# A second half-batch of banded attention moved to TensorE blocks, and the low parts of the first weights moved off TensorE

## The chip, the cores and the metric

The kernel runs on one core of a Trainium2 chip. Its time is the time that the device takes for one execution, in microseconds (us). The engines are named as the profile names them: PE is TensorE (PEld its weight loads), DVE is VectorE, ACT is ScalarE, POOL is GpSimd, SP is SyncE, which here issues most transfers (DMA).

## What is computed

An attention layer (4 batches, 8 heads, 576 tokens, head size 64) is followed by two feed-forward layers on its 2304 x 512 output, all in float32:

```python
q_d = q.reshape(B, H, Sd, factor, D).mean(axis=3)      # factor 4: also k_d, v_d
out_d = sm_attn(q_d, k_d, v_d)                          # full softmax attention on 144 groups
out_up = np.repeat(out_d, factor, axis=2)
mask = np.abs(pos[:, None] - pos[None, :]) < factor     # a band of 7 keys for each query
scores = np.where(mask, scale * np.matmul(q, k.transpose(0, 1, 3, 2)), -1000000000.0)
out_local = np.matmul(softmax(scores), v)               # softmax with 1e-9 in the divisor
x = (out_up + out_local).transpose(0, 2, 1, 3).reshape(B * S, H * D)
h = x @ w_in;  g = s * np.maximum(h, 0.0) ** 2 + b;  x = g @ w_out
h = x @ w_in2; g = h - np.tanh(h);                   out = g @ w_out2
```

## The kernel before

**Tiles and subs.** The first feed-forward layer works on 8 tiles of 288 tokens; tile j is the output of half a batch, which the code calls sub j (batch j // 2, half j % 2). For each tile and each of 16 slices f of the hidden layer PE has a group `hidden1(j, f)` of 12 matmuls into a bank of `hid`, and three slices later a group `output1(j, f)` of 12 matmuls into `acc`. Twelve, because every float32 operand is split in a high part (a rounded copy, made by ACT) and a low part (what the copy left out, made by subtraction), and high x high, low x high and high x low are summed over 4 blocks. The second layer has 6 tiles of 384 tokens and follows when the first is done.

**Weights.** w_in and w_out come in four 1 MB loads each (`load_w1a`, `load_w1b`). ACT makes the high parts (L1207). The low parts of the 32 pieces are made by POOL (L873), and for every fourth piece by PE: two matmuls, the raw piece by the identity and the high part by minus the identity, into a bank of `pa` (L1416, L1417), from which ACT copies the result (L1214).

**The band.** Sub 0 is computed in blocks by PE before the first tile ("dense": transposes L1429 and L1434, scores L1447, probabilities turned L1458, values L1475, with the masks and the softmax on DVE and ACT); it uses `hid` and `acc` while these are still free. Subs 1 to 7 are computed by DVE: products of queries and shifted keys (L988), their sums (L997), the softmax (L1029 to L1045), products with the values (L1058), a tree of sums (L1066 to L1076) into `oloc`. PE transposes `oloc` (L1529) into `pa`, and DVE adds the coarse attention `up` and writes `xraw` (L1107 for sub 1, L1118 for later ones). ACT copies the high part `xh` (L1320), POOL subtracts for the low part `xl` (L878). Two tiles of x are held, so that sub j is written when tile j - 2 has been read.

**The coarse attention** of each batch (group sums by POOL and DVE, transposes L1408, scores L1488, turned probabilities L1499, `weigh` L1516) runs beside the tiles, on PE between the large groups.

**What sets the order.** A planner in the kernel (`Plan`) lists all steps with costs, ranks and dependences, plays them once, and so fixes one order for each engine; the engines then run their lists and wait for each other by semaphores. All side work of PE during the tiles goes through the two banks of `pa` in turn ("fills"): a fill waits until the bank's last content has been taken out (`s_free0`, `s_free1`), and the large groups that stand behind it in PE's list wait too.

Of the kernel before, what the change touches and what calls it, by code (L numbers as in the profile page):

```python
# [13 lines left out]
P = 128  # L14
# [50 lines left out]
assert BSTEP1 * (BLOCKS - 1) + BQ == NS and DKEY % 3 == 0  # L65
# [7 lines left out]
def low_maker(f, half):  # L73

    return ("POOL", "POOL", "POOL", "PE")[(f + half) % 4]
# [106 lines left out]
def plan():  # L182
# [14 lines left out]
    for f in range(FT):  # L197
        for half in range(2):
            after = [(("load_w1a", "load_w1b")[half], f // WGROUP)]
            if half and f >= WGROUP:  # L200
                after.append(("dense_values", NPAIR - 1))
            o.add("ACT", act(512), (2, f + 3 * half) if f + 3 * half > 3 else (1, 0, 5), ("w1_high", f, half), after)
            maker = low_maker(f, half)
            if maker == "PE":
                o.add("PE", 1.1, (0, 9, f), ("w1_rest", f, half), [("w1_high", f, half)], 0.5, fills=True)
                o.add("ACT", act(512), (0, 9, f), ("w1_low", f, half), [("w1_rest", f, half)],
                      empties=("w1_rest", f, half))
            elif maker == "DVE":
                o.add("DVE", add(512), (0, 0, 9), ("w1_low", f, half), [("w1_high", f, half)])
            else:  # L210
                o.add("POOL", pool(512), (1, 0, NLOAD + f + 3 * half), ("w1_low", f, half), [("w1_high", f, half)])


    o.add("SP", 2.4, (0, 0, 0, 0), ("load_dense_keys",), kbytes=700)
    o.add("SP", 1.8, (0, 0, 0, 1), ("load_dense_queries",), kbytes=600)
    o.add("SP", 3.0, (1, 0, 0), ("load_dense_values",), kbytes=700)
    o.add("POOL", 3.0, (0, 1), ("dense_mask",))
    for a in range(NPAIR):
        o.add("PE", 1.0, (0, 0, 30 + 0), ("dense_turn", a), [("load_dense_keys",), ("load_dense_queries",), ("identity",)]
# [3 lines left out]
        o.add("ACT", 0.8, (1, 0, 30 + 0), ("dense_queries", a), [("dense_turn", a)] + ring)  # L223
        o.add("PE", 1.5, (0, 0, 30 + 1), ("dense_scores", a), [("dense_keys", a), ("dense_queries", a)]
# [8 lines left out]
        o.add("PE", 2.4, (0, 0, 30 + 3), ("dense_values", a), [("dense_place", a), ("load_dense_values",)]  # L233
              + {1: [("dense_keys", 3)], 2: [("dense_queries", 3)], 3: [("dense_add", 0)]}.get(a, []))
        o.add("DVE", 0.55, (0, 0, 0), ("dense_add", a), [("dense_values", a), ("place_up", 0, a)])

# [4 lines left out]
    for b in range(BATCH):  # L241
        for n in range(NLOAD):
# [5 lines left out]
                  kbytes=384 if n < 6 else 160)  # L248
# [10 lines left out]
        for n in range(6):  # L259
# [4 lines left out]
            o.add("ACT", 0.75, (1, b, n), ("place_columns", b, n), [("transposes", b, n)],  # L264
                  empties=("transposes", b, n))
        for i in range(2 * NPAIR):
# [3 lines left out]
            if b == 0 and qh:  # L270
                after.append(("dense_add", NPAIR - 1))
            o.add("PE", 0.3, (0, b, 6 + 2 * i), ("scores", b, i), after, lead(b), fills=True)
# [4 lines left out]
            o.add("ACT", 1.0, (1, b, 6 + 2 * i), ("score_exp", b, i), after, empties=("scores", b, i))  # L277
            o.add("DVE", 0.2, (0, b, i), ("score_inverse", b, i), [("score_exp", b, i)], .8 if b else 0.6)
            o.add("ACT", 0.64, (1, b, 7 + 2 * i), ("score_scale", b, i), [("score_inverse", b, i)])
# [5 lines left out]
            o.add("PE", 0.3, (0, b, 7 + 2 * i), ("turn_probs", b, i), after, lead(b), fills=True)  # L285
            o.add("ACT", 0.34, (1, b, 8 + 2 * i), ("place_probs", b, i), [("turn_probs", b, i)],
                  empties=("turn_probs", b, i))
            if b == 0 or qh:
                w = i if b == 0 else hp
                after = [("place_probs", b, i), ("group_sums", b, 7 + 2 * hp)]  # L290
                if b:
                    after.append(("add_up", b * NSUB - 1, NPART - 1))
                o.add("PE", 0.4, (0, b, 8 + 2 * i), ("weigh", b, w), after, lead(b), fills=True)
                o.add("ACT", 0.22, (1, b, 9 + 2 * i), ("place_up", b, w), [("weigh", b, w)], empties=("weigh", b, w))


    for s in range(1, SUBS):
        b = s // NSUB
        for i, (kind, loads, kbytes) in enumerate((("load_queries", 4, 600), ("load_keys", 4, 1000),
                                                   ("load_values", 4, 1000))):  # L300
            user = "value_products" if kind == "load_values" else "key_products"
            rank = (0, b, 2 * (s % NSUB) + (i == 2), i) if s > 1 else (2, (1, 1, 4)[i], i)
            o.add("SP", 0.6 * loads, rank, (kind, s), [(user, s - 1, len(UNITS) - 1)] if s > 1 else [], kbytes=kbytes)
        for a, (h2, t0, nt) in enumerate(UNITS):
            o.add("DVE", add(nt * BAND * HD), (1, s, a), ("key_products", s, a),
                  [("load_queries", s), ("load_keys", s)] + ([("score_inverse", 0, NPAIR - 1)] if s == 1 else []),
                  takes="prod")
            o.add("DVE", dve(nt * BAND * HD), (1, s, a), ("key_sums", s, a),
                  [("key_products", s, a)] + ([("band_exp", s - 1)] if s > 1 and a == 0 else []), gives="prod")
        o.add("DVE", 0.95, (1, s, 4), ("band_max", s), [("key_sums", s, len(UNITS) - 1)] + (  # L310
            [] if s > 1 else [("masks",)]))
        o.add("ACT", 0.32, (0, b, s), ("band_exp", s),
              [("band_max", s)] + ([("value_products", s - 1, len(UNITS) - 1)] if s > 1 else []))
        o.add("DVE", 1.0, (0, s, 5), ("band_norm", s), [("band_exp", s)], .6)
        for a, (h2, t0, nt) in enumerate(UNITS):
            after = [("band_norm", s), ("load_values", s)]
            if s > 1 and a == 0:
# [1323 lines left out]
```

## Time and profile before

| what | value |
|---|---|
| median of 3 runs | 942.22 us (941.83 to 943.9) |
| the profiled execution, its own time | 940.56 us |
| its span in the trace | 938.5 us |
| mean granted TensorE clock | 0.987 of full speed |
| busy: PE, DVE, ACT, POOL | 96%, 56%, 46%, 34% |
| first matmul of tile 0, of tile 1, of tile 2 | 50.70, 125.59, 187.75 us |
| first matmul of the second layer | 534.44 us |
| read from memory, written | 55.40 MB, 9.44 MB |

Times in the trace count from the start of the span. The chain of waits follows the work that ended last back from the end, at each step to what released it. A row of a timeline has the start, the length, the engine, the line, the operation, the output and inputs by the program's names, the shape, and in brackets the idle time just before and what ended it.

### The profile page before, as it was taken

How to read it: one execution, taken by the hardware profiler on the slowest of the kernel's cores; microseconds unless marked ns; L12 is line 12 of the kernel's file. 1: busy time of each engine (PE TensorE's matmuls, PEld its weight loads, DVE VectorE, ACT ScalarE, POOL GpSimd, SP SyncE). 2: the span in 40 equal slices, each digit the busy share in tenths (PEclk: the TensorE clock that was granted, in tenths of full speed). 3: DMA queues.
4: the chain of work that ended last, by engine and by line, in shares of the span. 5: the costliest groups of instructions: out<-in, count | busy, mean ns of one | idle time of the engine just before them, and what ended most of it. 6: DMA issues, size and time to landing. Idle time of an engine off the chain costs nothing.

```text
span 938.5 us, 15072 instructions
## 1 busy us (share of the span) xinstructions
PE 897.9 (96%) x5763; PEld 836.5 (89%) x5763; DVE 522.8 (56%) x641; ACT 432.0 (46%) x1096; POOL 319.3 (34%) x298
## 2 busy tenths in 40 slices
PE   5798999998999899999999999999999999999997
PEld 4576899998999899999999999999999999999996
DVE  4779979999898999982002452332322323322321
ACT  3777485555655575536546642322322323222221
POOL 6678867997369942533222100000000000000000
PEclk9798999999999999999999999999999999999999
DMA  8992242443334331002113600100200200100101
GB/s 227 264 285 78 75 110 68 111 106 96 68 102 114 105 69 43 27 1 94 34 38 132 227 14 1 56 13 1 68 1 1 68 1 0 35 1 1 34 1 34
DMA packets 41785, 65.81 MB, mean 70 GB/s; under 512 B 10932, under 2 KB 22770, under 8 KB 41714
## 3 DMA queue, kind: packets, MB, share of 16 engines
q1 hardware_dynamic: 40466, 63.28, 24.5%
q10 hardware_dynamic: 1248, 1.57, 0.6%
q8 instruction: 46, 0.75, 0.3%
q14 instruction: 25, 0.20, 0.1%
HBM read 55.40 MB, written 9.44 MB: 69 GB/s over the span
## 4 chain that ended last, share of the span: by engine, by line
PE 76%; DVE 12%; issue 3%; ACT 3%; DMA 3%; SPq 2%; DVEq 0%; ACTq 0%
PE acc L1606 21%; PE hid L1588 21%; PE hid L1549 16%; PE acc L1569 15%; DVE prod L1058 3%; DMA wb_raw<-in_moe_w_out_dram 3%; DVE prod L1066 2%; DVE prod L1071 2%; DVE oloc L1076 1%; PE pa L1488 1%; DVE sc L997 1%; ACT pc L1250 1%; PE pa L1516 1%; SPq L748 1%; DVE own L1008 1%
## 5 line engine op out<-in xcount | busy, mean ns | idle before, releaser
L887 POOL TENSOR_TENSOR gl<-relu,gh 128x288 fp32r<-128x288 f32 x128 | 133.0, 1041 | 179.1 <-PE acc L1569 141.4
L1569 PE MATMUL acc<-gh,wbh 128*128 128x288 f32 (+1 forms) x512 | 155.9, 305 | 0.2 <-ACT ystage L1347 0.2
L1549 PE MATMUL hid<-xh,wah 128*128 128x288 f32 x512 | 154.7, 304 | 1.1 <-POOL wal L873 1.1
L1143 DVE TENSOR_TENSOR gdif<-hid,tanh 128x384 f32<-128x384 f32 x96 | 53.5, 557 | 182.8 <-ACT tanh L1370 182.8
L1569 PE MATMUL acc<-gl,wbh 128*128 128x288 f32 (+1 forms) x512 | 152.0, 297 | 0.0
L1569 PE MATMUL acc<-gh,wbl 128*128 128x288 f32 (+1 forms) x512 | 151.8, 296 | 0.0
L1549 PE MATMUL hid<-xh,wal 128*128 128x288 f32 x512 | 150.4, 295 | 0.0
L1549 PE MATMUL hid<-xl,wah 128*128 128x288 f32 x512 | 146.8, 294 | 0.0
L1370 ACT ACTIVATE tanh<-hid 128x384 f32<-128x384 f32 x96 | 47.2, 491 | 186.9 <-PE hid L1588 186.9
L1588 PE MATMUL hid<-x2h,wah 128*128 128x384 f32 x384 | 129.0, 336 | 0.8 <-DVE gdif L1143 0.8
L1588 PE MATMUL hid<-x2h,wal 128*128 128x384 f32 x384 | 129.0, 336 | 0.0
L1588 PE MATMUL hid<-x2l,wah 128*128 128x384 f32 x384 | 128.9, 336 | 0.0
L1329 ACT ACTIVATE relu<-hid 128x288 f32<-128x288 f32 x128 | 52.3, 408 | 144.7 <-PE hid L1549 129.5
L1606 PE MATMUL acc<-wbl,g2h 128*128 128x512 f32 x288 | 112.6, 391 | 0.0
L1606 PE MATMUL acc<-wbh,g2l 128*128 128x512 f32 x288 | 112.4, 390 | 0.0
L1606 PE MATMUL acc<-wbh,g2h 128*128 128x512 f32 x288 | 112.2, 390 | 0.0
L1549 PEld LDWEIGHTS hid<-xh,wah 128*128 128x128 f32 x512 | 96.4, 188 | 4.4 <-issue 1.4
L1569 PEld LDWEIGHTS acc<-gh,wbh 128*128 128x128 f32 x512 | 97.1, 190 | 2.7 <-issue 1.1
L1569 PEld LDWEIGHTS acc<-gh,wbl 128*128 128x128 f32 x512 | 97.0, 190 | 0.7
L1569 PEld LDWEIGHTS acc<-gl,wbh 128*128 128x128 f32 x512 | 97.0, 189 | 0.0
L1549 PEld LDWEIGHTS hid<-xh,wal 128*128 128x128 f32 x512 | 96.2, 188 | 0.7
L1549 PEld LDWEIGHTS hid<-xl,wah 128*128 128x128 f32 x512 | 94.9, 188 | 0.0
(133 smaller groups left out, 1591.5 us busy)
## 6 DMA issues: line engine op xcount, KB each, us to landing
wa_raw<-in_moe_w_in_dram SPq DMA_DIRECT2D x8, 1024.0 KB, 8.6
wb_raw<-in_moe_w_out_dram SPq DMA_DIRECT2D x8, 1024.0 KB, 11.4
kl<-in_k_dram SPq DMA_DIRECT2D x27, 240.0 KB
vl<-in_v_dram SPq DMA_DIRECT2D x27, 240.0 KB
x2T<-ystage SPq DMA_DIRECT2D x8, 576.0 KB, 3.1
x2raw<-x2T SPq DMA_DIRECT2D x6, 768.0 KB, 4.5
own<-in_q_dram SPq DMA_DIRECT2D x11, 384.0 KB
ql<-in_q_dram SPq DMA_DIRECT2D x28, 144.0 KB, 3.7
```

Source lines behind the costliest of these rows:

```text
L748: sp.dma_start(dval[0:BK, i, :, :], dram(v, BKEY0[i] * HD, [[HD, BK], [HSTEP, HEADS], [1, HD]])).then_inc(s_dval, 16)
L887: g.tensor_tensor(out=gl[:, turn % LRING1, 0:NS], in0=relu[:, f % 2, :], in1=gh[:, turn % GRING1, 0:NS].bitcast(F32), op=ALU.subtract).the ...
L1058: ve.tensor_tensor(prod[:, 0:nt, :, :], vv, pv, ALU.mult).then_inc(s_mul, 1)
L1066: ve.tensor_tensor(prod[:, 0:nt, 0:3, :], prod[:, 0:nt, 0:3, :], prod[:, 0:nt, 3:6, :], ALU.add).then_inc(s_tree, 1)
L1071: ve.tensor_tensor(pairs, pairs, others, ALU.add).then_inc(s_tree, 1)
L1143: ve.tensor_tensor(gdif[:, f % 2, :], hid[:, f % 2, 0:N2], tanh[:, f % 2, :], ALU.subtract).then_inc(s_dif, 1)
L1329: sc.activation(r, hid[:, f % 2, 0:n], ACT.Relu).then_inc(s_relu, 1)
L1370: sc.activation(tanh[:, f % 2, :], hid[:, f % 2, 0:N2], ACT.Tanh).then_inc(s_tanh, 1)
L1549: one = pe.matmul(dst, w[:, d, cols], x[:, j % XRING, d, :], start=i == 0, stop=i == len(products) - 1)
L1569: one = pe.matmul(acc[:, d, n], w[:, f, cols], g[:, turn % ring, n], start=(f == 0 and p == 0), stop=(f == FT - 1 and p == 2))
L1588: one = pe.matmul(hid[:, f % 2, 0:N2], w[:, d, f * P:(f + 1) * P], x[:, j % 2, d, :], start=(d == 0 and p == 0), stop=(d == KT - 1 and p = ...
L1606: one = pe.matmul(acc[:, i, :], g[:, f % GRING2, i * P:(i + 1) * P], w[:, f, :], start=(f == 0 and p == 0), stop=(f == FT - 1 and p == 2))
```

## The change

Sub 1 is now computed in blocks by PE as well ("late"), for four pairs of heads. Its loads take the place of sub 1's loads of queries, keys and values in SP's list: rows of 64 numbers (256 bytes), as for sub 0, where the loads before had runs of 576 and 960 numbers. For each pair PE has six fills: keys turned, queries turned, scores, probabilities turned in two parts, values. All go through the two banks of `pa`, and DVE and ACT take each out. Two of the 24 fills stand before tile 0, the others between the groups of tile 0. The late buffers lie where the band's buffers lie, so DVE's first band product (now of sub 2) and its loads wait for the last late steps. x of tile 1 is split pair by pair as it is finished.

PE makes no low parts of weights any more: of the pieces from the fourth turn on, DVE makes every other one and POOL the rest (`turn_of` is f + 3 x half, half 1 being w_out, and is also the order in which ACT makes the high parts). Several costs, ranks and leads of the planner are changed, and the mask of the blocks has a third part.

```diff
+LKEY0 = [BSTEP1 * i for i in range(BLOCKS - 1)] + [DKEY - BK]
+LPARTS = [(0, 3), (3, 2)]
+SB = NSUB
 def low_maker(f, half):
-    return ("POOL", "POOL", "POOL", "PE")[(f + half) % 4]
+    return ("POOL", "DVE")[(f + half) % 2] if turn_of(f, half) >= 3 else "POOL"
+def turn_of(f, half):
+    return f + LAG1 * half
...
-    lead = lambda b: 3 if b else 0.0
+    lead = lambda b, late=False: 3 if b > 1 else 1.5 if b else 1.0 if late else 0.0
...
-            o.add("SP", 0.6, (2, 2 * g + 3 * i), (kind, g), after, kbytes=680)
+            o.add("SP", 0.6, (2, 2 * g + 3 * i), (kind, g), after, kbytes=620)
...
+            o.add("DVE", add(512), (0, 0, 24), ("w1_low", f, half), [("w1_high", f, half), ("dense_add", NPAIR - 1)])
...
+    for i, (kind, kbytes) in enumerate((("load_late_keys", 600), ("load_late_queries", 590), ("load_late_values", 870))):
+        o.add("SP", (2.4, 1.8, 3.0)[i], (2, (1, 1, 4)[i], i), (kind,), kbytes=kbytes)
+    for a in range(NPAIR):
+        o.add("PE", 0.35, (0, 0, 20), ("late_turn", 1, a), [("load_late_keys",)] + first, late, fills=True)
+        o.add("DVE", 0.45, (0, 0, 20), ("late_keys", a), [("late_turn", 1, a)] + ring, 0.3, empties=("late_turn", 1, a))
+        o.add("PE", 0.35, (0, 0, 20), ("late_turn", 0, a), [("load_late_queries",)] + first, late, fills=True)
+        o.add("ACT", 0.85, (-1, 0, 20), ("late_queries", a), [("late_turn", 0, a)] + ring, empties=("late_turn", 0, a))
+        o.add("PE", 1.0, (0, 0, 21), ("late_scores", a), [("late_keys", a), ("late_queries", a)] ..., late, fills=True)
+        o.add("DVE", 1.6, (0, 0, 21), ("late_max", a), [("late_scores", a)] ..., 0.3, empties=("late_scores", a))
+        o.add("ACT", 0.5, (-1, 0, 21), ("late_exp", a), [("late_max", a)])
+        o.add("DVE", 1.2, (0, 0, 22), ("late_norm", a), [("late_exp", a)], 0.3)
+        for part, (i0, n) in enumerate(LPARTS):
+            o.add("PE", 0.11 * n, (0, 0, 22), ("late_probs", a, part), [("late_norm", a)] ..., late, fills=True)
+            o.add("ACT", 0.1 + 0.13 * n, (-1, 0, 22), ("late_place", a, part), [("late_probs", a, part)] ...)
+        o.add("PE", 0.9, (0, 0, 23), ("late_values", a), [("late_place", a, 1), ("load_late_values",), ...], late, fills=True)
+        o.add("DVE", 0.45, (0, 0, 19), ("late_add", a), [("late_values", a)], 0.3, empties=("late_values", a))
...
-    for s in range(1, SUBS):
+    for s in range(SB, SUBS):
...
+                after = [("late_values", NPAIR - 1) if kind == "load_values" else ("late_turn", 0, NPAIR - 1)]
...
+                if s == SB and a == 0:
+                    r, m = bank("late_values", NPAIR - 1)
+                    ve.wait_ge(s_full[r], m)
```

**ACT, just before the first tile.** `wah` and `wbh` are the high parts of w_in and w_out, `s_wa1`, `s_wb0` and so on the loads that they wait for (the number is that of the load of four slices), `xh` the high part of x, `s_dadd` sub 0's last additions, `dpT` sub 0's turned probabilities. Before:

```order
L1207 ACTIVATE wah<-wa_raw 128x4x128 [waits s_wa0]
L1207 ACTIVATE wbh<-wb_raw 128x512 [waits s_wb0]
L1207 ACTIVATE wah<-wa_raw 128x4x128 [waits s_wa1]
L1320 ACTIVATE xh<-xraw 128x288 [waits s_dadd]
L1214 ACTIVATE wbl<-pa 128x512 [waits s_full0]
L1214 ACTIVATE wal<-pa 128x4x128 [waits s_full1]
L1329 ACTIVATE relu<-hid 128x288 [waits s_h]
```

and after:

```order
L1353 ACTIVATE wah<-wa_raw 128x4x128 [waits s_wa1]
L1472 ACTIVATE xh<-xraw 128x288 [waits s_dadd]
L1343 ACTIVATE dpT<-acc 66x512 [waits s_dprob,s_dout]
L1345 ACTIVATE dpT<-acc 66x128
L1353 ACTIVATE wbh<-wb_raw 128x512 [waits s_wb1,s_dout]
L1472 ACTIVATE xh<-xraw 128x288 [waits s_dadd]
L1353 ACTIVATE wah<-wa_raw 128x4x128 [waits s_wa1]
L1353 ACTIVATE wbh<-wb_raw 128x512 [waits s_wb1]
L1353 ACTIVATE wah<-wa_raw 128x4x128 [waits s_wa2]
L1311 ACTIVATE lqT<-pa 64x5x60 [waits s_full1,s_lzero]
```

A high part from the second load of w_out (`s_wb1`) now stands ahead of the last `xh` of tile 0; the copies of PE's low parts are gone.

**PE, after the second `output1` group of tile 0.** `pc` and `pT` belong to the coarse attention, `lkT`, `lqT` and `lkey` to the late blocks. Before:

```order
L1516 MATMUL pa<-pT,vd 64x72 [waits s_free0,s_sums]
L1516 MATMUL pa<-pT,vd 64x72 x3
L1516 MATMUL pa<-pT,vd 64x72 [waits s_free1,s_sums]
L1516 MATMUL pa<-pT,vd 64x72 x3
L1416 MATMUL pa<-wb_raw,ident 128x512 [waits s_w1high,s_minus,s_free0]
L1417 MATMUL pa<-wbh,minus 128x512
L1416 MATMUL pa<-wa_raw,ident 128x512 [waits s_w1high,s_minus,s_free1]
L1417 MATMUL pa<-wah,minus 128x512
```

and after:

```order
L1698 MATMUL pa<-ident,pc 72x72 [waits s_pc,s_free0]
L1698 MATMUL pa<-ident,pc 72x72 x3
L1608 MATMUL pa<-lkT,lqT 128x66 [waits s_free1,s_free0]
L1608 MATMUL pa<-lkT,lqT 128x66 x4
L1597 MATMUL pa<-ident,lkey 128x97 [waits s_free0]
L1597 MATMUL pa<-ident,lkey 128x97 x2
L1748 MATMUL hid<-xh,wah 128x288 [waits s_relu,s_w1vlow]
```

The first pair's scores and the second pair's keys stand where the low parts stood, and a large group follows at once.

**DVE, where sub 2's band begins.** The first product of sub 2 is the row with `ql,kl`. Before:

```order
L1071 TENSOR_TENSOR prod<-prod 128x4x2x64 [waits s_tree]
L1076 TENSOR_TENSOR oloc<-prod 128x4x64 [waits s_tree]
L988 TENSOR_TENSOR prod<-ql,kl 128x2240 [waits s_red,s_kl,s_ql]
L997 TENSOR_REDUCE sc_72<-prod 128x35 [waits s_mul,s_bexp]
L1107 TENSOR_TENSOR xraw<-pa,up 128x4x16 [waits s_full1]
```

and after:

```order
L1065 TENSOR_TENSOR xraw<-pa,up 128x288 [waits s_full0,s_free1]
L1138 TENSOR_TENSOR own<-own 128x6x64 [waits s_stage1]
L1141 TENSOR_TENSOR ks<-own 128x192 [waits s_vpairs]
L1065 TENSOR_TENSOR xraw<-pa,up 128x288 [waits s_full0,s_free0]
L1118 TENSOR_TENSOR prod<-ql,kl 128x2240 [waits s_kl,s_ql,s_full0]
L1065 TENSOR_TENSOR xraw<-pa,up 128x288 [waits s_full0,s_free1]
```

It followed the last sums of sub 1, and now follows the third of the four late additions and waits (`s_full0`) for the values of the fourth pair on PE.

## Rows read from the trace of the kernel before

**Rows 1.** The page: PE's busy time, share and instructions, with the other engines'.

```profile
PE 897.9 (96%) x5763; PEld 836.5 (89%) x5763; DVE 522.8 (56%) x641; ACT 432.0 (46%) x1096; POOL 319.3 (34%) x298
```

**Rows 2.** The page: shares of the chain that ended last, by engine.

```profile
PE 76%; DVE 12%; issue 3%; ACT 3%; DMA 3%; SPq 2%; DVEq 0%; ACTq 0%
```

**Rows 3.** Windows: length; busy PE, PEld, DVE, ACT, POOL; clock, DMA share, GB/s.

```profile
50.70:125.59 74.89, 66.57 (x459) 59.57 (x457) 69.18 (x73) 51.79 (x144) 61.80 (x44) 0.95 0.46 128
125.59:187.75 62.16, 61.25 (x476) 58.25 (x475) 54.51 (x51) 39.67 (x121) 46.38 (x41) 1.00 0.42 109
...
427.37:478.64 51.27, 51.27 (x389) 51.27 (x387) 5.24 (x10) 27.75 (x64) 15.97 (x20) 1.00 0.18 59
```

**Rows 4.** Waits of PE from 50.7 to 125.6: in total, times, longest.

```profile
PE pa L1529 <- DVE oloc L1076: 4.7, 2, 3.7
PE pa L1488 <- DVE xraw L1107: 1.2, 1, 1.2
```

**Rows 5.** Windows of 10 us, columns as in rows 3.

```profile
0.00:10.00 10.00, 0.00 (x0) 0.00 (x0) 2.94 (x6) 1.59 (x2) 6.71 (x20) 1.00 0.79 180
...
80.00:90.00 10.00, 6.30 (x36) 5.04 (x35) 9.90 (x6) 7.85 (x17) 10.00 (x6) 0.90 0.20 68
90.00:100.00 10.00, 10.00 (x56) 8.85 (x55) 9.76 (x17) 3.06 (x8) 4.42 (x5) 0.76 0.26 86
```

**Rows 6.** Timeline of PE in tile 0: two low parts, and six transposes of sub 1.

```profile
80.05 1.02 PE L1416 MATMUL pa<-wb_raw,ident 128*128 128x512 f32 x2
...
81.15 1.02 PE L1416 MATMUL pa<-wa_raw,ident 128*128 128x512 f32 x2
...
108.74 0.85 PE L1529 MATMUL pa<-ident,oloc 128*128 128x128 f32 x6 [0.97 <-DVE oloc L1076]
```

**Rows 7.** Timeline of PE before tile 0: one pair of sub 0's blocks, step by step.

```profile
18.18 0.69 PE L1429 MATMUL hid<-ident,dkey 97*128 97x97 f32 x3
18.67 0.68 PE L1434 MATMUL hid<-ident,dqry 96*128 96x96 f32 x3
...
26.95 1.23 PE L1447 MATMUL acc<-dkT,dqT 128*128 128x66 f32 x10
28.01 0.71 PE L1458 MATMUL acc<-ident,dprob 128*66 128x128 f32 x5
...
29.14 0.80 PE L1475 MATMUL acc<-dpT,dval 66*64 66x57 f32 x20
```

**Rows 8.** Weights: the chain's first load, two issues, and their times to landing.

```profile
25.76 17.72 DMA wb_raw<-in_moe_w_out_dram
25.29 0.43 SPq L776 DMA_DIRECT2D wa_raw<-in_moe_w_in_dram  x1
37.80 0.54 SPq L788 DMA_DIRECT2D wb_raw<-in_moe_w_out_dram  x1
wa_raw<-in_moe_w_in_dram SPq DMA_DIRECT2D x1, 1024.0 KB, 14.8
wb_raw<-in_moe_w_out_dram SPq DMA_DIRECT2D x1, 1024.0 KB, 19.1
```

**Rows 9.** Timelines of ACT and POOL around the first matmul of tile 0.

```profile
43.51 0.63 ACT L1207 ACTIVATE wbh<-wb_raw 128x512 fp32r<-128x512 f32 x1 [1.16 <-DMA wb_raw<-in_moe_w_out_dram]
48.23 0.44 ACT L1320 ACTIVATE xh<-xraw 128x288 fp32r<-128x288 f32 x1 [0.35 <-DVE xraw L948]
50.16 0.80 POOL L878 TENSOR_TENSOR xl<-xraw,xh 128x288 fp32r<-128x288 f32 x1
```

**Rows 10.** Timelines of DVE and POOL: sub 2 from its first product to its x.

```profile
108.73 2.87 DVE L988 TENSOR_TENSOR prod<-ql,kl 128x2240 f32<-128x2240 f32 x1
114.10 1.87 DVE L1107 TENSOR_TENSOR xraw<-pa,up 128x64 f32<-128x64 f32 x10
177.00 0.40 DVE L1118 TENSOR_TENSOR xraw<-pa,up 128x128 f32<-128x128 f32 x1
179.96 4.91 POOL L878 TENSOR_TENSOR xl<-xraw,xh 128x288 fp32r<-128x288 f32 x4
```

More of the change, by code:

```diff
@@ L195, in plan @@
             after = [("dense_values", NPAIR - 1)] if i and 2 * g >= FT // WGROUP else []
-            o.add("SP", 0.6, (2, 2 * g + 3 * i), (kind, g), after, kbytes=680)
[L197 to L211, printed above, removed]
@@ L214, in plan @@
-    o.add("SP", 2.4, (0, 0, 0, 0), ("load_dense_keys",), kbytes=700)
-    o.add("SP", 1.8, (0, 0, 0, 1), ("load_dense_queries",), kbytes=600)
-    o.add("SP", 3.0, (1, 0, 0), ("load_dense_values",), kbytes=700)
+            o.add("SP", 0.6, (2, 2 * g + 3 * i), (kind, g), after, kbytes=620)
+    for f, half in sorted(itertools.product(range(FT), range(2)), key=lambda one: turn_of(*one)):
+        turn = turn_of(f, half)
+        after = [(("load_w1a", "load_w1b")[half], f // WGROUP)]
+        if half and f >= WGROUP:
+            after.append(("dense_values", NPAIR - 1))
+        if turn > 1:
+            after.append(("place_up", 0, NPAIR - 1))
+        o.add("ACT", act(512), (2, turn) if turn > 2 else (1, 0, 5), ("w1_high", f, half), after)
+        maker = low_maker(f, half)
+        if maker == "PE":
+            o.add("PE", 1.1, (0, 9, f), ("w1_rest", f, half), [("w1_high", f, half), ("hidden1", 0, 1)], 0.5, fills=True)
+            o.add("ACT", act(512), (0, 9, f), ("w1_low", f, half), [("w1_rest", f, half)],
+                  empties=("w1_rest", f, half))
+        elif maker == "DVE":
+            o.add("DVE", add(512), (0, 0, 24), ("w1_low", f, half), [("w1_high", f, half), ("dense_add", NPAIR - 1)])
+        else:
+            o.add("POOL", pool(512), (1, 0, NLOAD + turn), ("w1_low", f, half), [("w1_high", f, half)])
@@ L263, in plan @@
             o.add("PE", 0.35, (0, b, n), ("transposes", b, n), after, lead(b), fills=True)
-            o.add("ACT", 0.75, (1, b, n), ("place_columns", b, n), [("transposes", b, n)],
+            o.add("ACT", 0.75, (0 if b else -1, b, n), ("place_columns", b, n), [("transposes", b, n)],
                   empties=("transposes", b, n))
@@ L270, in plan @@
             if b == 0 and qh:
-                after.append(("dense_add", NPAIR - 1))
-            o.add("PE", 0.3, (0, b, 6 + 2 * i), ("scores", b, i), after, lead(b), fills=True)
+                after.append(("hidden1", 0, 0))
+            o.add("PE", 0.3, (0, b, 6 + 2 * i), ("scores", b, i), after, lead(b, qh), fills=True)
             o.add("DVE", 0.46, (0, b, i), ("score_max", b, i), [("scores", b, i)], .8 if b else 0.5)
@@ L1287, in scalar_program @@
                 r, m = bank("weigh", b, n)
-                if b and n == 0:
+                if b > 1 and n == 0:
                     for part in range(NPART):
                         ra, ma = bank("columns", b * NSUB - 1, part)
+                        sc.wait_ge(s_free[ra], ma)
+                elif b and n == 0:
+                    for a in range(NPAIR):
+                        ra, ma = bank("late_values", a)
                         sc.wait_ge(s_free[ra], ma)
@@ L1313, in scalar_program @@
                     sc.wait_ge(s_dadd, d + 1)
+                elif j == 1:
+                    ra, ma = bank("late_values", d)
+                    sc.wait_ge(s_free[ra], ma)
                 elif d == 0:
```

325 lines of the change are left out of this document (234 added, 91 removed).

## The prediction

> **What bounds the kernel now.** I read four views, from wide to narrow. The page's busy shares: PE is at work for 96% of the span, and no other engine comes near [rows 1]. The chain that ended last: 76% PE, 12% DVE, the rest small [rows 2]. So an edit counts by what it does to PE's list, or to a place where PE waits for another engine. The windows by tile then say where such places are. A tile that is nothing but its 32 large groups takes 51.27, so a group costs 1.60 [rows 3]. Between the first groups of tile 0 and tile 1 stand 29 groups, 46.4 by that price; the stretch took 74.89 with PE busy for 66.57 [rows 3]. Tile 1 took 62.16 with PE busy for 61.25: nearly all of its surplus is side work, not waits.
>
> Tile 0's surplus of 28.5 splits as follows. Waits 74.89 - 66.57 = 8.3: 4.7 of them for `oloc` and 1.2 for the additions to `xraw`, both of sub 1's band on DVE [rows 4], 2.4 others. Lost clock: the granted clock was 0.90 and 0.76 in the two slices that hold and follow PE's longest wait, 3.7 us [rows 4, 5], that is 10 x (0.10 + 0.24) = 3.4. Low parts by PE: six in this stretch, 1.10 from one to the next [rows 6], 6.6. Sub 1's nine transposes: six took 0.85 [rows 6], so 1.3. That leaves 28.5 - 8.3 - 3.4 - 6.6 - 1.3 = 8.9 of other side work, which stays.
>
> **The change part by part: tile 0.** It loses the 5.9 of waits for sub 1's band, the 3.4 of clock that followed the longest of them, the 6.6 and the 1.3. It gains four pairs of blocks. Sub 0's pair shows the price on PE: turns 0.49 (18.18 to 18.67) and as much again for the queries, scores 1.06 (26.95 to 28.01), probabilities 0.71, values 0.80 [rows 7], together 3.55; four are 14.2. Two of the 24 fills, both turns of the first pair, stand ahead of tile 0, so 13.2 fall in it. On PE's work alone the exchange costs 13.2 - 7.9 = 5.3; it pays only by the waits and the clock.
>
> How long PE waits in the new tile 0 is not in the trace, since late fills take turns with coarse fills in the same two banks, and each step of a pair goes PE, DVE or ACT, PE. The lower bound is the 2.4 of other waits that the old tile had; the upper is half of the 22 fills waiting 1 us each beside those, near 14, where 1.2 is the one wait that the trace has for a bank emptied by DVE [rows 4]. I take 5.2: 1.6 at the start; 1.5 at banks, where a coarse copy on ACT stands ahead of a late one; 2.1 where the second pair's last probabilities wait for a DVE that stands in the next batch's group sums, and those for their loads. The new tile is then 46.4 + 8.9 + 13.2 + 5.2 = 73.7, against 74.89: **-1.2**, between -4.0 and +7.6.
>
> DVE has the room in sum: it loses sub 1's whole band, and takes 15 low parts of 512 columns. At 2.87 per 2240 [rows 10] one is 0.66, together 10. POOL is rid of some pieces and had been at work through all of 80 to 90 [rows 5]. I cost both at nothing; if DVE makes a low part late, the group that reads it waits, which is within the 14.
>
> **The start of tile 0.** The two low parts that PE made ahead of it go, some 2.2. This gives nothing: ACT's list now has a `wbh` of the second load of w_out ahead of tile 0's last `xh`. Behind that wait are queued the `xh`, three more high parts and the copy of the late queries, which holds a bank of `pa`; for the `xh` POOL waits with `xl`, and PE with the first group. So the start hangs on when that load lands. Before, the first load of w_out landed at 25.76 + 17.72 = 43.5 and the second at 37.80 + 19.1 = 56.9 [rows 8], 13.4 later, with a load of w_in and 0.98 MB of values between them. The second of w_in landed at 25.29 + 14.8 = 40.1 [rows 8], so 1 MB of weights takes 3.4 at that point. The values between were thus 13.4 - 6.8 = 6.6. Now 0.34 MB less lie ahead of the first load of w_out (1.1 us: 42.4), and 0.68 MB of late values between the two. At the weights' rate that is 2.2 and the landing at 51.4; at the old values' rate 4.5 and 53.7. I take the middle, 52.5, as rows of 256 bytes have a price in the first slice only: 180 GB/s at a share of 0.79, 228 GB/s when busy [rows 5], between the two. From the landing: high part 0.63, `xh` 0.44, `xl` 0.80 [rows 9], a last matmul 0.13: the first group ends at 54.5. It ended one group's price after its start, at 50.70 + 1.6 = 52.3 [rows 3]: **+2.2**. Bounds: without the hold, POOL's `xl` would stay at 50.16 to 50.96 [rows 9] and the group could end 0.7 earlier; with nothing saved ahead of the loads and the high price, 54.8 and +4.5.
>
> PE is idle for some us ahead of this start, with two turns in it. What such idling costs in clock stands in the slices behind the 3.7 wait: 0 to 2.4 [rows 5]. I take half, **+1.2**.
>
> The Trainium skill (DMA: Bandwidth & Descriptors, Specifications) says that transfers below 512 bytes miss the line rate because the engine reads, modifies and writes. The late rows are of 256 bytes where runs of 2304 and 3840 stood, so this rule speaks against the change. The trace agrees in part: 228 GB/s against the weights' 308 (1.05 MB in 3.4).
>
> **Tile 1.** x of tile 1 is done pair by pair with the late additions, so it no longer waits for DVE's last sums. What is late next is sub 2. DVE's first product of it began at 108.73, which is 16.9 before tile 1; now it waits for the values of the fourth pair, with the last late addition and the whole chain of sub 2 queued behind, and PE has these values three groups and about 1 us of small fills before tile 1: 5.8. From the first product to the last low part sub 2 took 76.1 (108.73 to 184.87) [rows 10]. Of it go sub 1's additions, 1.87, and one product of sub 3 that stood ahead of the additions, 2.87 [rows 10]: 71.4, so tile 2 could start 65.6 after tile 1 instead of 62.16. That is +3.4 if DVE's idle time in this stretch stays, 62.16 - 54.51 = 7.6 [rows 3], and 0 if half of it goes. I take the middle, **+1.7**; the upper bound is +5, if the loads of sub 2 come late too. They are queued on SP: queries and keys behind the last turn, values behind the last late values, and loads of the next batch behind each. Sub 3 onwards I cost at nothing, with +-2 for another order: PE in tile 6 has no wait at all [rows 3].
>
> **The sum.** +2.2 + 1.2 - 1.2 + 1.7 = +3.9. The profiled execution took 940.56 (span 938.5 and 2.1 around it) and would take 944.5; the median of the runs stands 1.7 above it, and 942.2 + 3.9 gives **946.1**.
>
> **The rivals.**
> First, faster: the loads land early enough or ACT is not held, and the fills find their banks free. Then the start is -0.7, the clock nothing, tile 0 at its lower bound -4.0, tile 1 unchanged: -4.7, 937.5. For it speaks that PE's old waits in tile 0 were of one kind and that kind is gone [rows 4]; against it, that the new list puts a load ahead of the last `xh`. It decides at the landing: before some 49.5 the hold costs nothing.
> Second, no change: the hold is there (+2.2, clock 1.2), but the banks are as free as in the first rival and tile 2 finds its x ready: 3.4 - 4.0 = -0.6, 941.6.
> Third, the banks become the bound: 11 us of waits behind them instead of 3.6, +7.4 on the sum, 953.5. For it speaks that ACT and DVE were at work for 7.9 and 9.9 of 10 us in 80 to 90 [rows 5]; against it, that half of this DVE time was the band that goes.
> Fourth, the small rows: each moved twice, 154 GB/s instead of 308, makes 1.9 MB cost 6.2 more than at the weights' rate, so the load lands at 57.6 and the start is +7.3, in all +9.0, 951.2. The 228 GB/s of the first slice [rows 5] speak against the full size. The skill's sentence above is about this.
>
> **How the numbers follow.** My forecast 0.33, faster 0.30, no change 0.18, banks 0.13, small rows 0.06. What a measurement of this kernel can tell from no change is about 0.2%, 1.9 us. So slower has 0.33 + 0.13 + 0.06 = 0.52, the same 0.18, faster 0.30. Cases of both signs hold much of it: the forecast's own range is 942.5 to 950 (tile 0's waits from 3 to 8, the landing from 51.4 to 53.7). The whole range takes in the first rival with 1 us more, and the third: 936.5 to 953.5.
>
> **What would show it.** Right: an idle time on ACT ahead of that `wbh`, ended by the second load of w_out near 52.5; a first group of tile 0 that ends near 54.5; no wait of PE for `oloc` in tile 0, and tile 1 at about 128; DVE's first product of sub 2 some 6 us before tile 1; a wait of PE for `xl` or `oloc` ahead of tile 2, and tile 1 near 64; a second layer that starts near 538.3. Wrong: a first group that ends by 52, which is the first rival's start; waits of PE for `pa` beyond 8 us in tile 0, which is the third; a granted clock below 0.8 after 60, which would add a cost that I have only at the start; or a time shift that arises behind tile 2, where I have none.

## The result

| | before | after |
|---|---|---|
| median of 5 runs | 942.22 us | 936.07 us |
| ratio to before, 95% interval | | 0.9932 (0.9908 to 0.9956) |
| the profiled execution, its span | 940.56, 938.5 | 937.84, 935.8 |
| first matmul of tile 0, 1, 2, 3, 4 | 50.70, 125.59, 187.75, 251.34, 309.39 | 53.73, 125.84, 187.89, 252.58, 309.11 |
| first matmul of the second layer | 534.44 | 532.33 |

The kernel became 6 us faster; 3.9 slower was forecast, and the time lies 0.4 below the range. The two spans differ by 2.7 only: the profiled execution of after was the longest of its five. Two more traces of the same kernel, called the second (the run after_again) and the third (after_c) below, have spans of 933.5 both, 5.0 below that of before. In those two measurements the medians differ by 4.9 and 6.9.

The page of after, busy times and the chain by engine, answer to [rows 1, 2]. PE is busier by 8 us in a shorter span, DVE's part of the chain fell from 12% to 10%, PE's rose from 76% to 84%:

```profile
PE 906.3 (97%) x5894; PEld 847.2 (91%) x5894; DVE 496.6 (53%) x647; ACT 436.4 (47%) x1107; POOL 294.8 (32%) x292
...
PE 84%; DVE 10%; ACT 3%; issue 2%; DMA 1%; SPq 0%; DVEq 0%; ACTq 0%
```

The windows by tile (columns as in [rows 3]) of after:

```profile
53.73:125.84 72.11, 70.27 (x586) 65.87 (x586) 46.31 (x74) 52.23 (x141) 41.03 (x42) 1.00 0.38 110
125.84:187.89 62.05, 61.75 (x480) 59.01 (x479) 56.63 (x56) 41.09 (x130) 34.84 (x33) 1.00 0.36 96
187.89:252.58 64.69, 61.51 (x457) 57.55 (x455) 60.09 (x61) 40.82 (x127) 52.03 (x43) 1.00 0.43 105
```

and tiles 0 and 1 of the second trace:

```profile
51.60:122.85 71.25, 69.30 (x587) 64.71 (x586) 46.19 (x74) 52.44 (x142) 39.28 (x39) 0.97 0.41 120
122.85:185.63 62.78, 61.96 (x480) 58.99 (x479) 58.25 (x56) 41.04 (x130) 37.30 (x35) 1.00 0.35 95
```

Tile 0 took 72.11 and 71.25 for 74.89 (71.59 in the third trace), although the start of it still holds a stretch at the long matmul time (below). PE has 127 records more in it and idles for 1.8 and 2.0 instead of 8.3. DVE fell from 69.18 to 46.31. What PE waited for in tile 0 of after, in total, times and longest, is three waits, where [rows 4] had 4.7 and 1.2 for sub 1's band:

```profile
PE pa L1687 <- DVE lkT L1022: 1.1, 1, 1.1
PE pa L1632 <- DVE lkT L1022: 0.5, 1, 0.5
PE pa L1715 <- ACT lqT L1311: 0.2, 1, 0.2
```

Each window's change against before, in us:

| window | forecast | after | second trace | third trace |
|---|---|---|---|---|
| start of tile 0, clock there included | +3.4 | +3.0 | +0.9 | +1.0 |
| tile 0 | -1.2 | -2.8 | -3.6 | -3.3 |
| tile 1 | +1.7 | -0.1 | +0.6 | -0.1 |
| tiles 2 to 4 | 0 | -2.1 | -2.1 | -1.9 |
| tiles 5 to 7, second layer and end | 0 | -0.8 | -0.8 | -0.7 |
| span | +3.9 | -2.7 | -5.0 | -5.0 |

**The start.** In ACT's timeline of after, answer to [rows 9], the high part that waits for the second load of w_out starts at 52.90, and its idle time was ended by sub 0's last values on PE, not by the load:

```profile
52.90 0.63 ACT L1353 ACTIVATE wbh<-wb_raw 128x512 fp32r<-128x512 f32 x1 [1.51 <-PE acc L1674]
53.47 0.44 ACT L1472 ACTIVATE xh<-xraw 128x288 fp32r<-128x288 f32 x1
```

In the second trace it is the load, and in the third the load too, at 53.31:

```profile
52.37 0.63 ACT L1353 ACTIVATE wbh<-wb_raw 128x512 fp32r<-128x512 f32 x1 [3.10 <-DMA wb_raw<-in_moe_w_out_dram]
52.91 0.43 ACT L1472 ACTIVATE xh<-xraw 128x288 fp32r<-128x288 f32 x1
```

What I had not seen is that sub 0 itself is done later: its last values start at 51.54 in after (40.92 before). The coarse steps of the first batch now go ahead of its third pair on ACT: DVE has that pair ready at 33.2, and ACT takes its exponential at 40.02. That exponential in ACT's timelines of before, of after, and of the changed kernel with the planner's old numbers (`old_numbers`, below):

```profile
30.19 0.48 ACT L1190 ACTIVATE dprob<-dprob 128x330 f32<-128x330 f32 x1
```

```profile
40.02 0.47 ACT L1336 ACTIVATE dprob<-dprob 128x330 f32<-128x330 f32 x1
```

```profile
30.29 0.47 ACT L1334 ACTIVATE dprob<-dprob 128x330 f32<-128x330 f32 x1
```

With the old numbers sub 0's last values start at 41.89 again; the kernel before with the new numbers alone (`new_numbers`) has 39.59 for the exponential and 49.58 for these values. So it is the planner's numbers that set sub 0 back.

And ahead of tile 0 PE runs at different speed in different executions. The ten matmuls of a pair's scores, in the timeline of PE of after and then of the second trace:

```profile
29.03 2.24 PE L1646 MATMUL acc<-dkT,dqT 128*128 128x66 f32 x10
```

```profile
27.46 1.23 PE L1646 MATMUL acc<-dkT,dqT 128*128 128x66 f32 x10
```

The second is the time of [rows 7]. The first is near twice it, the lower of the two clock levels (1.2 against 2.4 GHz), and in after this goes on into tile 0. Three matmuls of PE's timeline, each of 288 columns, the first two 0.24 from the start of the next, the last at the end of this stretch:

```profile
54.12 0.44 PE L1748 MATMUL hid<-xh,wal 128*128 128x288 f32 x1
...
61.72 0.43 PE L1748 MATMUL hid<-xh,wal 128*128 128x288 f32 x1
61.96 0.33 PE L1748 MATMUL hid<-xl,wah 128*128 128x288 f32 x1
```

Later they take 0.29 each and 0.133 from start to start. Up to 62 stand twenty large matmuls and four scores (0.48 for 0.24): 20 x 0.107 + 4 x 0.24 = 3.1 us lost. In the second trace the short time is back after twelve large matmuls and part of the scores, 12 x 0.107 + 0.4 = 1.7 lost. Before, the two low parts on PE ran without a pause from 46.47 on, and the first matmul of tile 0 already took 0.29:

```profile
46.47 2.04 PE L1416 MATMUL pa<-wb_raw,ident 128*128 128x512 f32 x2 [3.71 <-ACT wbh L1207]
...
50.70 0.29 PE L1549 MATMUL hid<-xh,wah 128*128 128x288 f32 x1
```

The mean granted clock of a whole execution tells the two kinds apart. Of the thirteen traces kept here without added transposes, five have PE at the long time until 52 or later (scores 2.24); their mean clock reads 0.994 to 0.998, since the lower clock ahead of the first change is not in it. In the other eight PE first comes to the short time by 30.2, and the mean reads 0.978 to 0.991. By this number six of the sixteen measured executions of the changed kernel stayed at the long time, with 937.2 us in the mean, and ten did not, with 935.2. Of the 53 executions of the kernel before that were measured beside the experiments none did (0.982 to 0.991).

**Sub 2.** DVE's first product of it, behind the third late addition and PE's last late values, in DVE's timeline of after:

```profile
115.17 0.46 DVE L1065 TENSOR_TENSOR xraw<-pa,up 128x288 f32<-128x288 f32 x1 [3.08 <-PE pa L1632]
120.02 2.98 DVE L1118 TENSOR_TENSOR prod<-ql,kl 128x2240 f32<-128x2240 f32 x1 [4.40 <-PE pa L1632]
```

It starts 5.8 ahead of tile 1, as forecast. POOL's low parts of tile 2's x end at 191.0, 71.0 after it (76.1 in [rows 10], 71.4 forecast), and PE waits for them in the first group of tile 2 (timelines of POOL and PE):

```profile
186.14 4.86 POOL L951 TENSOR_TENSOR xl<-xraw,xh 128x288 fp32r<-128x288 f32 x4
```

```profile
190.30 0.40 PE L1748 MATMUL hid<-xl,wah 128*128 128x288 f32 x1 [0.91 <-POOL xl L951]
191.05 0.40 PE L1748 MATMUL hid<-xl,wah 128*128 128x288 f32 x1 [0.35 <-POOL xl L951]
```

### The profile page after: what moved, and what is told of

It reads as the page before. It is cut to its first block, busy times and chain, and to the rows that moved or that the text cites. A ratio compares the mean times of both kernels' runs of the same rounds, so it can differ in the third digit from the quotient of the medians.

```text
span 935.8 us, 15370 instructions
## 1 busy us (share of the span) xinstructions
PE 906.3 (97%) x5894; PEld 847.2 (91%) x5894; DVE 496.6 (53%) x647; ACT 436.4 (47%) x1107; POOL 294.8 (32%) x292
## 4 chain that ended last, share of the span: by engine, by line
PE 84%; DVE 10%; ACT 3%; issue 2%; DMA 1%; SPq 0%; DVEq 0%; ACTq 0%
PE acc L1805 21%; PE hid L1787 21%; PE acc L1768 17%; PE hid L1748 17%; DVE prod L1190 2%; PE pa L1687 2%; DVE prod L1198 1%; DVE prod L1203 1%; PE pa L1715 1%; DVE sc L1127 1%; DVE prod L1118 1%; PE acc L1646 1%; PE pa L1698 1%; ACT ystage L1499 1%; PE pa L1560 1%
## 5 line engine op out<-in xcount | busy, mean ns | idle before, releaser
L960 POOL TENSOR_TENSOR gl<-relu,gh 128x288 fp32r<-128x288 f32 x128 | 124.5, 975 | 195.3 <-PE acc L1768 142.9
```

The source lines that it names most:

```text
L960: g.tensor_tensor(out=gl[:, turn % LRING1, 0:NS], in0=relu[:, f % 2, :], in1=gh[:, turn % GRING1, 0:NS].bitcast(F32), op=ALU.subtract).the ...
```

## Experiments

Kernels that were measured together share the runs of the kernel before.

### One half alone

`low_only`, on the kernel before:

```diff
-    return ("POOL", "POOL", "POOL", "PE")[(f + half) % 4]
+    return ("POOL", "DVE")[(f + half) % 2] if f + 3 * half >= 3 else "POOL"
```

> The kernel before with one edit: no low parts of weights by PE; from the fourth turn on DVE makes every other piece and POOL the rest. Sub 1's band stays on DVE. Theory A (the two halves need each other): PE loses six low parts of 1.10 in tile 0, 6.6, but DVE, busy for 69.2 of 74.9 us in tile 0, gets about 10 us more, so sub 1's oloc comes later and PE waits for it; tile 0 stays within 3 us of 74.9 and the time within 3 us of 942. Rival B (the low parts are the gain, the band costs as much as it frees): tile 0 loses 6.6 and the time falls to about 936.

`band_only`, on the changed kernel (the eight low parts go first in the two banks):

```diff
-    return ("POOL", "DVE")[(f + half) % 2] if turn_of(f, half) >= 3 else "POOL"
+    return ("POOL", "POOL", "POOL", "PE")[(f + half) % 4]
-                o.add("PE", 1.1, (0, 9, f), ("w1_rest", f, half), [("w1_high", f, half), ("hidden1", 0, 1)], 0.5, fills=True)
+                o.add("PE", 1.1, (0, 0, 0), ("w1_rest", f, half), [("w1_high", f, half)], 0.5, fills=True)
-                o.add("ACT", act(512), (0, 9, f), ("w1_low", f, half), [("w1_rest", f, half)],
+                o.add("ACT", act(512), (-1, 9, f), ("w1_low", f, half), [("w1_rest", f, half)],
```

> The changed kernel with the low parts made as before (every fourth piece by PE, through the two banks), sub 1 in blocks on PE. Theory A: PE has the eight low parts of 1.10 again beside the blocks, so tile 0 is longer than in the changed kernel by 6.6 to 8.8 and the time is 943 to 945; but the first low parts may warm PE's clock for the start. Rival B (low parts are the gain): 942. Rival C (the band is the gain, the low parts had been hidden): 936 to 938.

`after_again` is the changed kernel itself.

> The changed kernel once more, as the measure for the edits of it and for a second trace: 936 +- 1.5. The first trace's span was 2.7 below the span of before where the medians differ by 6.1. If this is the spread of executions, the second trace differs from the first by some us at places that vary; if the tiles start at the same times within 0.5, the difference stays open.

Measured together: low_only 945.8, ratio 1.0043 (1.0027 to 1.0059); band_only 949.96, 1.0096 (1.0077 to 1.0115); after_again 936.58, 0.9949 (0.9933 to 0.9966). Each half alone makes the kernel slower, by 4 and 8, and both together make it faster by 5. Theory A holds in its direction, both sizes were too small. The windows of tile 0 of low_only and of band_only:

```profile
45.02:134.56 89.54, 70.10 (x461) 60.69 (x460) 84.02 (x92) 57.41 (x170) 65.59 (x53) 0.84 0.50 136
```

```profile
55.75:131.58 75.83, 73.44 (x601) 65.59 (x600) 30.69 (x60) 54.69 (x145) 42.18 (x43) 1.00 0.31 87
```

In low_only tile 0 starts 5.7 earlier, as the two low parts ahead of it are gone, and then takes 14.7 more: PE idles for 19.4, with DVE at work for 84 of 89.5. Its three longest waits in tile 0:

```profile
PE pa L1488 <- DVE xraw L1107: 5.2, 1, 5.2
PE pa L1408 <- DVE ks L1011: 3.0, 1, 3.0
PE hid L1549 <- POOL xl L878: 2.6, 1, 2.6
```

In band_only DVE has room (30.69) and PE waits little, but works for 3.2 more in tile 0 than in after; it starts 2.0 later, and tiles 1 and 2 take 64.48 and 69.77. Against after its span is 13.1 longer. Tile 0 holds 3.7 of that: six low parts of 1.10 more, and 3.1 of clock less, as PE is at the short time from 54.9 on. Tiles 1 and 2 hold 7.5; the longest wait there is in tile 2 and not for a low part:

```profile
PE pa L1687 <- DVE xraw L1232: 4.7, 1, 4.7
```

So a half alone has its price together with the order that the planner makes for it. What low_only shows is that DVE can't take them beside sub 1's band: it was at work for 84 of 89.5 us there. That PE's low parts were cheap while PE waited for DVE anyway is argued, not shown: the kernel before with all low parts on POOL was not run.

### The planner's numbers

`new_numbers` is the kernel before with the new costs, ranks, leads and the new conditions of the high parts, `old_numbers` the changed kernel with the old ones. Their core:

```diff
-    lead = lambda b: 3 if b else 0.0
+    lead = lambda b, late=False: 3 if b > 1 else 1.5 if b else 1.0 if late else 0.0
-            o.add("ACT", 1.0, (1, b, 6 + 2 * i), ("score_exp", b, i), after, empties=("scores", b, i))
+            o.add("ACT", 1.0, (0 if b else -1, b, 6 + 2 * i), ("score_exp", b, i), after, empties=("scores", b, i))
...
+            after.append(("place_up", 0, NPAIR - 1))
```

> The kernel before with the planner's new costs, ranks and leads alone (of loads, of sub 0's steps, of the coarse steps of the first batches, and the high parts behind the first four place_up); sub 1 stays on DVE, PE makes its eight low parts. Rival J (the new numbers are the gain, since they also changed the order from tile 2 on, where the changed kernel's two traces gained 2.1 and 2.3): 936 to 939. Theory A (the gain is in tile 0, by what DVE and PE no longer do): tile 0 keeps its waits for oloc and its low parts, 940 to 946.

> The changed kernel with the planner's old costs, ranks and leads of those steps, and with sub 1 in blocks and no low parts on PE. Theory A with theory G (the blocks and the low parts are the gain, the new numbers only trade the start against tile 0): the start is earlier than in the changed kernel by some 2, tile 0 longer by as much or more, 935 to 941. Rival J (the new numbers are the gain): 942 or more, the kernel before.

Measured: new_numbers 943.67, 1.0009 (0.9994 to 1.0025); old_numbers 935.9, 0.9938 (0.9919 to 0.9956), measured together. The numbers are not the gain, by either kernel; theory A holds. They trade one stretch for another, as the windows of tiles 0 and 1 of old_numbers show:

```profile
46.82:116.81 69.99, 67.26 (x585) 63.87 (x583) 44.80 (x74) 52.41 (x141) 40.54 (x39) 0.98 0.46 139
116.81:182.53 65.72, 62.92 (x485) 59.27 (x483) 60.27 (x58) 42.06 (x133) 35.87 (x37) 1.00 0.37 92
```

It starts 4.8 ahead of the second trace and gains 1.3 more in tile 0, but loses 2.9 in tile 1, 2.3 in tile 2 (66.96) and 1.1 in tiles 3 and 4; the second layers start at 530.04 and 530.03.

### Who makes the low parts

`pool_all`, on the changed kernel:

```diff
-    return ("POOL", "DVE")[(f + half) % 2] if turn_of(f, half) >= 3 else "POOL"
+    return "POOL"
```

> The changed kernel with all 32 low parts on POOL (DVE makes none, PE none). If DVE's share matters (theory A: in tile 0 POOL had been at work through whole slices before, and groups wait for low parts): POOL gets 15 more of about 1.3 us, tile 0's groups wait for them, tile 0 is 3 to 10 us longer, 939 to 946. Rival I (POOL has the room): within 1 us of the changed kernel.

Measured 939.58, 0.9964 (0.9951 to 0.9977), where the changed kernel had 0.9932, 0.9949 and 0.9929: some 1 to 3 slower than it, though its interval meets two of these three. If DVE's share matters, it is not where I put it: tile 0 takes 71.58, as in after, and the loss stands in tiles 1 and 2 (62.05 and 64.69 in after).

```profile
122.68:186.14 63.46, 62.41 (x481) 58.87 (x479) 60.55 (x57) 40.94 (x129) 47.89 (x43) 1.00 0.37 96
186.14:253.81 67.67, 64.54 (x461) 60.94 (x459) 62.94 (x64) 41.58 (x128) 51.81 (x44) 0.95 0.42 105
```

In tile 2 PE idles for 3.1, as in after (3.2). It works for 3.0 more, as the granted clock is at half from 189.9 to 196.7; it fell among four waits for `xl` of 2.0 together (two of 1.3 in after, where the clock stayed at 1.00).

### The start: the hold, the order, the clock

`xh_swap`: after the planner's play, ACT's last `xh` of tile 0 is put ahead of the high part that waits for the load.

```diff
+    acts = o.order["ACT"]
+    high, last_x = acts.index(("w1_high", WGROUP, 1)), acts.index(("x_high", 0, KT - 1))
+    if high < last_x:
+        acts.insert(high, acts.pop(last_x))
```

> The changed kernel with one exchange in ACT's list: the last xh of tile 0 ahead of the high part of the second w_out load, nothing else moved. The prediction's step (the hold): the wait for that load delays the start by 2.2, so without it the start comes some 2 us earlier and the time is 934. Rival F, from the two traces of the changed kernel: sub 0's last addition ended at 53.4 and 51.3 and the load landed near 52.5, so the hold costs 0.5 to 2 in some executions and nothing in others; within 1 us of the changed kernel, 935.5 to 936.5.

`dense_first`: ACT's three steps of each of sub 0's pairs (queries, exponential, probabilities placed) get rank -1 for 1; the diff shows one.

```diff
-        o.add("ACT", 0.5, (1, 0, 30 + 1), ("dense_exp", a), [("dense_max", a)])
+        o.add("ACT", 0.5, (-1, 0, 30 + 1), ("dense_exp", a), [("dense_max", a)])
```

> The changed kernel with one number of the planner changed: ACT's steps of sub 0's blocks get the rank -1, that of the coarse steps of the first batch (it was 1, behind them). Theory G (the new ranks set sub 0 back: its third pair's exponential stands behind the coarse steps on ACT, its last values at 51.5 and 49.4 in the two traces, 40.9 before): the last values come 4 to 8 us earlier, tile 0 starts at 45 to 48, and as the tile behind it is bound by PE, most of it is kept: 930 to 932. Rival H (what is won at the start is lost in tile 0, which then waits for loads and DVE): 935 to 937.

`warm_first` and `warm_all`: transposes of the identity on PE, at the start alone and at eleven places (the line as in warm_all).

```diff
+                pe.transpose(bank[:, 0:P], ident[:, :], ident[:, :])
```

> The changed kernel with 24 transposes of the identity on PE while it waits for the first load, into a bank that is overwritten. In the trace of the changed kernel every matmul up to 61.9 takes twice the later time (288 columns 0.24 from start to start against 0.133), the first group of tile 0 too; before, the rows from 26 to 37 and from 49 on ran at the short time. Theory D (the clock at the start sets when sub 0 is done): with the short time from 10 on, PE's steps of sub 0 take half, the first group ends 2 to 6 us earlier, the time is 930 to 934. Rival E (the steps of sub 0 hang on DVE, ACT and loads, or the clock falls back in their gaps): within 1 us of the changed kernel, 935 to 937.

> The changed kernel with transposes of the identity at eleven places of PE's list ahead of tile 0 where it waited in the traces (24 at the start, 2 to 14 elsewhere, 92 in all), into banks that nobody reads then. The 24 at the start alone had brought PE to the short time for 1 us, and it fell back in the gaps. Theory D again: with the gaps filled PE keeps the short time until tile 0, the first group runs at 0.133 a matmul, and against the execution that stayed at the long time some 5 us are won: 931 to 934. Rival E: the steps hang on DVE and ACT, PE only waits for them at the short time; the first group is 1.3 faster and the time 934.5 to 936.

Measured: warm_first 935.63, 0.9934 (0.9916 to 0.9953), together with after_again, 0.9949; later and without the changed kernel beside them xh_swap 934.19, 0.9912 (0.9896 to 0.9928), dense_first 933.3, 0.9913 (0.9886 to 0.9941), warm_all 935.46, 0.992 (0.9904 to 0.9936). The intervals meet that of the changed kernel in the result (0.9908 to 0.9956); xh_swap's lies just below that of after_again (0.9933 to 0.9966).

dense_first moved the fourth pair's exponential on ACT (42.91 for 47.29 in after) and not the third's (39.84); tile 0 starts at 49.88. Its median hides two kinds of executions, told apart by the mean clock as above: two took 938.8 and 938.7, four 930.4 to 933.6. Against the changed kernel (937.2 and 935.2) that is 1.5 slower in the one kind and 2.7 faster in the other, so theory G is near where PE comes to the short time early, and rival H where it does not. These are few executions, sorted after the fact.

The clock: in warm_first the first turns run at the short time and the next pair's no longer, one gap of 0.39 further on; the timeline of PE:

```profile
10.09 0.41 PE L1588 MATMUL hid<-ident,dqry 96*128 96x96 f32 x3
10.89 0.68 PE L1583 MATMUL hid<-ident,dkey 97*128 97x97 f32 x3 [0.39 <-DVE dkT L982]
```

In warm_all PE holds the short time from 26.5 to 40.2 and in the first group of tile 0, yet that starts at 53.02, and with a wait of 2.3 for `lkT` behind the first group the clock falls again, to half from 57.2 to 60.6. From 9.4 to 26.5 and from 40.2 to 50.4 PE was at the long time in spite of the transposes, ten of which took 2.40 there; that they cost PE what the short time later wins fits this, but no run separates it. Theory D is not borne out: filling these eleven places did not hold PE at the short time up to tile 0.

The hold, on one chip:

> The kernel of the run xh_swap again (the last xh of tile 0 ahead of the high part that waits for the second w_out load), on one chip with the changed kernel. The prediction's hold: 1.5 to 2.5 below the changed kernel. Rival F (the hold costs only where sub 0 is done before the load lands): 0 to 1 below.

> The changed kernel, the measure for xh_swap_b: 935.5 to 937.5; a third trace, with the first matmul of tile 0 between 51.5 and 54 by the clock ahead of it.

Measured: xh_swap_b 935.75, 0.9936 (0.9919 to 0.9953), after_c 934.92, 0.9929 (0.9916 to 0.9941). Rival F: without the hold the kernel is not faster in the median. Three of the six executions of xh_swap_b are of the kind that stays at the long time, none of the five of after_c; of the other kind they took 934.1 and 934.8 in the mean, 0.6 apart. What the hold costs PE stands in the first group of tile 0: nothing in after; in the second trace two of its matmuls start 0.44 apart for 0.24, 0.2; in the third PE waits for `xh`, 1.26 for 0.24 from start to start, 1.0. The timelines of ACT and of PE of the third trace:

```profile
53.31 0.63 ACT L1354 ACTIVATE wbh<-wb_raw 128x512 fp32r<-128x512 f32 x1 [3.92 <-DMA wb_raw<-in_moe_w_out_dram]
```

```profile
54.33 0.61 PE L1749 MATMUL hid<-xh,wah 128*128 128x288 f32 x1 [0.81 <-ACT xh L1473]
```

In the trace of xh_swap `xh` is at 50.33, with no wait for the load:

```profile
50.33 0.44 ACT L1476 ACTIVATE xh<-xraw 128x288 fp32r<-128x288 f32 x1 [2.07 <-DVE xraw L1078]
52.04 0.63 ACT L1357 ACTIVATE wbh<-wb_raw 128x512 fp32r<-128x512 f32 x1 [1.27 <-DMA wb_raw<-in_moe_w_out_dram]
```

Against the second trace its second layer starts 1.6 earlier, but 1.0 of this is there when tile 0 starts (50.60 for 51.60), as sub 0's last values were 1.0 earlier: that is not the hold. In the trace of xh_swap_b sub 0's last values ended at 52.9, past the load, and its second layer starts at 532.09, with after's 532.33.

`dense_first_s5` adds to dense_first a lead of 4.0 for sub 5's turns, since PE waited 4.3 ahead of them in tile 4 of dense_first:

```profile
PE pa L1728 <- ACT pc L1396: 4.3, 1, 4.3
```

> The changed kernel with rank -1 for ACT's steps of sub 0's blocks, as in the run dense_first, and in addition a longer lead (4.0 for 2.5) for the turns of sub 5's result on PE, since in that run PE waited 4.6 in tile 4 ahead of them. Theory G: tile 4 is back at 64 and the time 2 to 5 below dense_first's 933.3, 928 to 931. Rival H: the wait turns up elsewhere, 932 to 935.

Measured 933.9, 0.9909 (0.988 to 0.9939). Rival H: tile 4 takes 68.67 (70.23 in dense_first, 63.92 in after), and the wait stands ahead of another fill instead:

```profile
PE pa L1687 <- ACT pc L1396: 4.2, 1, 4.2
```

In both the granted clock falls to half around the end of this wait, for 6.9 us in dense_first and 3.4 here, and PE works for 2.7 and 1.2 more in tile 4 than in after. Tile 0 does start at 46.21 here, and 74.55 for tile 0 gives 2.4 of it back. One execution of this run took 938.5, the five of the other kind 929.0 to 934.5. No version here is shown to be faster than the changed kernel; all but low_only, band_only and new_numbers are faster than the kernel before, clear of the noise.

## The prediction's steps

**Right: what tile 0 loses.** The waits for sub 1's band, the low parts and the clock behind the long wait are gone, as put down, and no wait for `oloc` is left in tile 0.

**Wrong, and the largest single term: the waits of the late fills.** The sum took 5.2 for PE's waits in tile 0 (bounds 2.4 to 14); after and the second trace have 1.8 and 2.0, below my lower bound, and the third 2.3, 0.8 of it for `xh`, which is the hold. Waits for banks behind ACT's copies came to 0.2 and 0.6, and the wait of the second pair's probabilities did not come about. With 72.11 - 46.4 - 8.9 - 1.8 - 3.1 of clock, 11.9 is left by difference for the blocks that I had at 13.2; with 71.25, 2.0 and 1.7 of the second trace it is 12.3. With the priced terms and these two sizes the tile would have been 46.4 + 8.9 + 11.9 + 1.8 = 69.0, -5.9, before any cost of the clock. The first rival, faster by 4.7, rested on that and had 0.30; that its 937.5 came near the median is in part luck, as its start of -0.7 and its clock of nothing did not come about, and the 2.1 of tiles 2 to 4 were not in it. This term alone does not turn the forecast's sign either: +3.9 - 3.2 = +0.7. The start and tiles 2 to 4, below, do.

**Right about the load, wrong about what the start hangs on.** I had the landing of the load at 52.5; ACT passed it at 52.37 in the second trace and 53.31 in the third. So the rival of the small rows, which put the landing at 57.6, is out; that transfers below 512 bytes miss the line rate (the Trainium skill, DMA: Bandwidth & Descriptors, Specifications) shows here at most as far as the middle between the bounds. But the start depends first on when sub 0 is done, which I left where it was, and that hangs on PE's clock and on the coarse steps ahead of it. The first group ended at 56.96, 55.19 and 56.13 (54.5 forecast, without the clock), and the start moved by +3.0, +0.9 and +1.0 for 3.4. The hold is hidden in one trace and cost PE 0.2 and 1.0 in the others, so +2.2 for it was too much. The two low parts that went, which I had at 2.2 ahead of tile 0, had taken 4.2 (46.47 to 50.70 before): they ran at the long time, behind a wait of 3.7; low_only, without them, starts 5.7 earlier.

**Half: the clock.** That it costs at the start was right; 3.1 in after and some 1.7 in the second trace, against 1.2 taken and 2.4 as the bound. What I missed is that this differs from one execution to the next. The Trainium skill (TensorE: Matmul & The Clock Gate, Part 1) says that how many matmuls of the same kernel run at the lower clock varies from run to run. The two traces agree in kind, with the short time first seen at 62.0 in tile 0 of one and at 25 to 35 already in the other.

**Right, but a tile later: sub 2.** 5.8 and 71.4 were met within 0.4. The cost showed as waits of 1.3 in tile 2's first group, not as +1.7 on tile 1.

**Wrong: nothing from tile 2 on.** Tiles 2 to 4 took 185.1 for 187.2, though tile 2 itself is longer. PE idles in tile 4 for 1.8 instead of 3.4 and has fewer records in tile 3. new_numbers has -2.3 in the same three tiles and old_numbers +1.3, which points at the new order, but low_only has -6.1 there with the old numbers, behind a tile 0 that is longer by 14.7. So these tiles also gain where tile 0 takes longer, and in the whole time the order is worth nothing (1.0009). What makes the 2.1 stays open.

**Where the 10 us between forecast and median went**, by the second trace: start 2.5, tile 0 2.4, tile 1 1.1, tiles 2 to 4 2.1, the rest 0.8, together 8.9; the last 1.1 is how the traced executions stand to the medians.

## What to carry to other kernels

Two changes that each move work onto the engine that the other one relieves must be priced together: alone they cost 4 and 8 us here, each with the order that the planner made for it, and together they gave 5 to 7. Work interleaved between long matmul groups had next to no waits here with the engines that empty its banks idle for a third of the tile (DVE at work for 46.31 of 72.11, ACT for 52.23), so a bound of "half of the fills wait" was far off; in low_only, with DVE at work for 84 of 89.5, PE idled for 19.4. By these two stretches the idle share of the emptying engines is the better guide. A reordered list can win the start and lose it two tiles later, so an order is judged by when the last common stage starts.

## What the hardware showed unexpectedly

The granted clock reads 1.00 in every window of after up to tile 0, while scores take 2.24 there instead of 1.23 and matmuls of 288 columns 0.24 instead of 0.133; in the second trace, where PE had come to the short time once, the window of 40 to 50 reads 0.50. In these traces the column thus reads 1.00 until the first change that it records, and ahead of that the matmul's own duration tells the level. The same program ran with either in different executions, and its first tile began at 53.73 in the one and at 51.60 and 51.73 in the others.
